# Seven block products for u in batches 3 to 6, relu in the gate, and kv loads issued after the spread of the roots

## The chip, the core and the metric

The kernel runs on one core of a Trainium2 chip. TensorE (PE) multiplies matrices, VectorE (DVE) and ScalarE (ACT) do the elementwise work, GpSimd (POOL) a little of it, and SyncE (SP) issues most of the transfers between HBM and the on-chip memory. Each engine works through its own list of instructions in order and is held by semaphores. The metric is the device time of one execution in microseconds (us).

## What is computed

Three layers follow one another, on 8 batches of 576 positions:

```python
kv = einsum('bhsd,bhse->bhde', k, v); out = einsum('bhsd,bhde->bhse', q, kv)      # 8 heads of 64
x = out / sqrt(mean(out*out) + 1e-6) * g_norm                                     # -> (8, 576, 512)
h = maximum(x @ w_in, 0); u, v = h[..., :512], h[..., 512:]
v_n = (v - mean(v)) / sqrt(var(v) + 1e-6)
gated = u * (einsum('ts,bsd->btd', w_spatial, v_n) + b_spatial)
y = gated @ w_out                                                                 # 512 -> 512
h = maximum(y @ w_in2, 0); c = conv over the positions, 3 taps per channel, of h  # 512 -> 1024
result = (h * sigmoid(c)) @ w_out2                                                # 1024 -> 512
```

## The kernel before

All matrices are fp32; a large product is made of three passes over operands that were split into a high part (rounded to fp32r) and a low part (the rest), so that each block of 128 rows of the contraction costs three matmuls. The program is written by hand, engine by engine; nothing schedules it. `w_out @ w_in2` is combined into one matrix at the start, so that y is never made. Two stages follow.

**Stage 1** (to about 408 us) has a body for each batch b. On PE its order is: the four tiles of v (`v_product`, L461, 12 matmuls of 512 columns each) and the rest tile (L487), between them the attention product o of batch b+1 (`o_product`, 16 matmuls); then the sum of squares for batch b+1 (`square_sum`), the kv product of batch b+2 (`kv_product`, L404), the product for u (`u_product`, L494: four output tiles m, each 2 x 12 matmuls of 288 columns), and the spatial product (`spatial_product`, L504: four tiles, each 28 matmuls of 288 columns). Every wait of PE is on a count of another engine's work: `s_vr` counts the relus of v (they free PSUM banks), `s_vlo` the low halves of the normalised v, `s_ur` the relus of u, `s_x` the split parts of the next batch's x, and `s_g` the gates. The tiles 0 and 1 of v of a batch start once three gates of the batch before are done (L467), the others after the fourth.

DVE's order in a body (`body`, L1138) is: for each of the five v tiles its statistics, scale and low part; a copy of half of kv; `inverse_root(b + 1)` (L1054), which makes the roots r of batch b+1 and ends at L1069; the last `v_lo`; `gate` 0 (L1133); `x_scale` of batch b+1 (L1071, four instructions); gate 1; `x_lo` (L1084, four and a rest); gate 2; gate 3; and four differences T of the gated values (`t_a`, `t_b`, `t_c`, L1185), which go to the operand scratch in HBM for stage 2. `x_scale` waits for `s_rB`.

SP sends the roots on their way (`spread_r`, L250): four small stores of r to HBM (L253), a wait for their landing, and two loads (L258) that spread them over all partitions into `rB` (sq_then_r in the trace). Then it waits for the kv product of batch b+2 and issues the load of k and v of batch b+3 (`load_kv`, L243), and then the stores of the gated values.

ACT does the relus (`v_relu`, `u_relu` L744), squares, square roots and high parts (`x_hi` L704, `v_hi`). In bodies 1 and 2 it also splits `w_out2`, and `wo2_store` (L818) sends the split half to HBM out of memory that it shares with stage 2.

**Stage 2** (from about 408 us) computes h in blocks by the scheme of seven products for a 2 x 2 block matrix product (`PRODUCTS`, L70), `in_product` (L608), with sums by DVE at L1285, and then the gate by the convolution and the last product.

Of the kernel before, what the change touches and what calls it, by code (L numbers as in the profile page):

```python
# [18 lines left out]
ALU = mybir.AluOpType  # L19
# [41 lines left out]

HI, LO = 0, 1
# [9 lines left out]
GROUPS = FT // 2  # L72
PER_BATCH = NPROD * GROUPS

# [6 lines left out]
def build(nc, q_T, kv_main_dram, kv_rest_dram, consts, w_in, w_sp_T, b_sp, w_out_T, w_in2, w_out2, wo2_dram, op_dram, r_dram, out):  # L81
    with ExitStack() as ctx:
# [104 lines left out]
        selT = sb("head_spread", [P, CH * MT, D])  # L187
# [36 lines left out]
        s_T, s_To = map(sem, ("s_T", "s_To"))  # L224
        s_go = [sem("s_go0"), sem("s_go1"), sem("s_go2")]
# [7 lines left out]
        s_odr = sem("s_odr")  # L233

# [7 lines left out]
        def _(sp):  # L242
# [78 lines left out]
            sp.wait_ge(s_u, B * MT)  # L321
# [81 lines left out]
        def _(pe):  # L403
# [100 lines left out]
            def spatial_product(b, m):  # L504
                if m == 0:
                    pe.wait_ge(s_vlo, (b + 1) * NT)
                    pe.wait_ge(s_ur, b * MT + 1)
                if m == 1:
                    pe.wait_ge(s_ur, b * MT + 2)
                if m == 2:  # L510
                    pe.wait_ge(s_ur, b * MT + 4)
# [3 lines left out]
                wide(GATE_PAIR[m], steps).then_inc(s_sp, 1)  # L515

            def body(b, ahead, two_ahead):
# [15 lines left out]
                for m in range(MT):  # L533
                    if m == 3 and two_ahead:
                        pe.wait_ge(s_kvd0, b + 3)
                        pe.wait_ge(s_kvd1, b + 3)
                    u_product(b, m, ahead)
# [3 lines left out]
                for m in range(MT):  # L541
                    spatial_product(b, m)
# [58 lines left out]
            body(0, True, True)  # L601
            with pe.Fori(1, B - 2) as b:
                body(b, True, True)
            body(B - 2, True, False)
            body(B - 1, False, False)

# [70 lines left out]
        def _(act):  # L677
# [26 lines left out]
            def x_hi(a, m):  # L704
                act.wait_ge(s_xm, a * MT + m + 1)
                if m == 0:
                    act.wait_ge(s_u, a * MT)
# [35 lines left out]

            def u_relu(b, m):  # L744
                act.wait_ge(s_u, b * MT + m + 1)
# [8 lines left out]
            def body(b, ahead, two_ahead):  # L754
# [18 lines left out]
                if two_ahead:  # L773
                    kv_copy(b + 2)
                u_relu(b, 0)
# [4 lines left out]
                if ahead:  # L780
# [9 lines left out]
                    for m in range(MT):  # L790
                        x_hi(b + 1, m)
                else:
# [111 lines left out]
            body(0, True, True)  # L904
            body(1, True, True)
            body(2, True, True)
# [559 lines left out]
```

## Time and profile before

| | us |
|---|---|
| median of 3 runs | 790.61 |
| lowest and highest run | 790.01, 791.25 |
| the profiled execution, its own time | 789.98 |
| its span in the trace | 788.0 |

Between the span and the own time of the profiled execution lie 2.0 us that the trace does not cover. The profile gives for every engine the busy time, for every group of instructions a mean duration, and for a wait who ended it. A row of the timeline has the start, the duration, the engine, the line of the source and the instruction, and in brackets the idle time ahead of it with what ended it. TensorE had its full clock in the whole span.

### The profile page before, as it was taken

The page shows a single profiled execution, that of the slowest core. Times are in us where ns is not written, and L with a number is a line of the kernel's source. Part 1 is how long each engine was busy: PE and PEld are TensorE (multiplying, and loading weights), DVE is VectorE, ACT ScalarE, POOL GpSimd, SP SyncE. Part 2 cuts the span into 40 slices and gives each one's busy share as a digit, 9 for nine tenths or more (in the row PEclk, how much of TensorE's full clock was granted, in tenths as well). Part 3 has the DMA queues.
Part 4 walks back from the last instruction along what each step waited for, and adds up shares of the span by engine and source line. Part 5 has one row for each costly group of instructions (what it writes and reads, how often), then busy time and mean ns, then how long its engine had stood idle before and what let it go on. Part 6 is the DMA issues. An engine that isn't in the chain of part 4 may idle for free.

```text
span 788.0 us, 15294 instructions
## 1 busy us (share of the span) xinstructions
PE 779.9 (99%) x5654; PEld 702.0 (89%) x5654; DVE 583.4 (74%) x1262; ACT 421.8 (54%) x753; POOL 29.4 (4%) x40
## 2 busy tenths in 40 slices
PE   9999999999999999999999999999999999999997
PEld 7679789798998979899999898998989899898986
DVE  3765785867577474757899989497985979689791
ACT  4664362644335253442457767375774757567562
POOL 4342000000000000000000000000000000000000
PEclk9999999999999999999999999999999999999999
DMA  9872629556252642213092212221021212102102
GB/s 325 306 254 67 245 92 296 208 193 233 76 209 86 195 150 61 106 46 99 23 364 74 106 42 105 68 104 56 7 109 58 105 53 101 57 14 105 54 0 67
DMA packets 35005, 96.92 MB, mean 123 GB/s; under 512 B 2738, under 2 KB 9106, under 8 KB 30228
## 3 DMA queue, kind: packets, MB, share of 16 engines
q1 hardware_dynamic: 33476, 90.09, 33.7%
q10 hardware_dynamic: 1488, 6.30, 2.1%
q8 instruction: 23, 0.38, 0.2%
q14 instruction: 18, 0.15, 0.1%
HBM read 66.11 MB, written 30.28 MB: 122 GB/s over the span
## 4 chain that ended last, share of the span: by engine, by line
PE 91%; DVE 3%; DMA 3%; ACT 1%; issue 1%; SPq 1%; ACTq 0%; DVEq 0%
PE ps L642 25%; PE ps L457 25%; PE ps L634 21%; PE ps L483 11%; PE ps L426 2%; PE ps L410 2%; PE ps L490 2%; PE ps L561 1%; DMA work<-w_out_T_dram 1%; DMA sq_then_r<-r_scratch 1%; PE ps L436 1%; DVE vrr L1115 0%; DVE h_and_sums L1285 0%; DVE t_then_s L1185 0%; PE ps L549 0%
## 5 line engine op out<-in xcount | busy, mean ns | idle before, releaser
L642 PE MATMUL ps<-w_in_split,v_hg_split 128*128 128x512 f32 x832 | 194.9, 390 | 0.0
L642 PEld LDWEIGHTS ps<-w_in_split,v_hg_split 128*128 128x128 f32 x832 | 155.7, 188 | 32.2
L457 PE MATMUL ps<-w_sp_split,v_hg_split 128*128 128x288 f32 x896 | 120.1, 295 | 0.0
L457 PEld LDWEIGHTS ps<-w_sp_split,v_hg_split 128*128 128x128 f32 x896 | 119.3, 188 | 0.0
L457 PE MATMUL ps<-x_operand_split,w_in_split 128*128 128x288 f32 x768 | 103.8, 296 | 0.0
L457 PEld LDWEIGHTS ps<-x_operand_split,w_in_split 128*128 128x128 f32 x768 | 102.1, 188 | 0.7 <-issue 0.2
L483 PE MATMUL ps<-w_in_split,x_operand_split 128*128 128x512 f32 x384 | 92.1, 393 | 1.6 <-DVE work L1136 1.6
L483 PEld LDWEIGHTS ps<-w_in_split,x_operand_split 128*128 128x128 f32 x384 | 71.1, 188 | 19.1 <-issue 3.1
L1285 DVE TENSOR_TENSOR h_and_sums<-h_and_sums,ps 128x288 f32<-128x288 f32 x160 | 68.4, 449 | 7.7 <-PE ps L634 7.2
L1136 DVE TENSOR_TENSOR work<-ps,work 128x576 f32<-128x576 f32 x32 | 24.0, 756 | 66.6 <-PE ps L457 66.5
L1285 DVE TENSOR_TENSOR h_and_sums<-work,ps 128x288 f32<-128x288 f32 x64 | 28.2, 450 | 46.8 <-PE ps L634 46.3
L634 PE MATMUL ps<-x_operand_split,w_combined 128*128 128x288 f32 x384 | 61.6, 295 | 0.0
L925 ACT ACTIVATE h_and_sums<-h_and_sums 128x576 f32<-128x576 f32 x64 | 43.4, 678 | 29.4 <-DVE h_and_sums L1285 28.7
L723 ACT ACTIVATE work<-ps 128x512 f32<-128x512 f32 x32 | 19.1, 597 | 74.1 <-PE ps L483 70.0
L634 PE MATMUL ps<-operand_more_split,w_combined_more 128*128 128x288 f32 x384 | 56.5, 295 | 0.3 <-DVE h_and_sums L1285 0.3
L634 PEld LDWEIGHTS ps<-x_operand_split,w_combined 128*128 128x128 f32 x384 | 54.7, 188 | 0.0
L634 PEld LDWEIGHTS ps<-operand_more_split,w_combined_more 128*128 128x128 f32 x384 | 52.9, 188 | 0.6 <-DVE h_and_sums L1285 0.6
L1328 DVE SCALAR_TENSOR_TENSOR work<-h_and_sums,const_cols,work 128x576 f32<-128x576 f32 x64 | 51.9, 812 | 0.3
L1322 DVE SCALAR_TENSOR_TENSOR work<-h_and_sums,const_cols,work 128x576 f32<-128x576 f32 x64 | 51.9, 811 | 0.0
L931 ACT ACTIVATE work<-h_and_sums,const_cols 128x576 f32<-128x576 f32 x64 | 49.7, 776 | 3.0
L1333 DVE TENSOR_TENSOR work<-h_and_sums,work 128x576 f32<-128x576 f32 x64 | 48.0, 750 | 0.3 <-ACT work L941 0.3
L752 ACT ACTIVATE work<-ps 128x576 f32<-128x576 f32 x32 | 20.8, 650 | 49.3 <-PE ps L457 49.2
(124 smaller groups left out, 1066.8 us busy)
## 6 DMA issues: line engine op xcount, KB each, us to landing
kv_raw<-kv_main_dram SPq DMA_DIRECT2D x8, 2048.0 KB, 11.8
q_raw<-q_T_dram SPq DMA_DIRECT2D x8, 1152.0 KB, 5.1
operand_scratch<-t_then_s SPq DMA_DIRECT2D x8, 1152.0 KB, 4.7
operand_raw<-operand_scratch SPq DMA_DIRECT2D x8, 1152.0 KB, 5.5
sq_then_r<-r_scratch SPq DMA_DIRECT2D x14, 576.0 KB, 7.0
operand_scratch<-work SPq DMA_DIRECT2D x24, 288.0 KB, 2.7
operand_more_raw<-operand_scratch SPq DMA_DIRECT2D x8, 864.0 KB, 7.2
w_out_split_scratch<-v_hg_split ACTq DMA_DIRECT2D x2, 2048.0 KB, 13.9
```

The lines of the kernel that those rows point to most:

```text
L457: last = pe.matmul(pair[bank][:, c, :], st, mo[:, c * HALF:(c + 1) * HALF], start=(n == 0), stop=(n == len(steps) - 1))
L483: last = pe.matmul(PS[:, V_BANK[i], 0:F1], XG[:, a, m, i * P:(i + 1) * P], WA[:, w, m, F1:2 * F1], start=(n == 0), stop=(n == len(steps) - 1))
L634: last = pe.matmul(PS[:, n % 8, 0:HALF], st, mo, start=(i == 0), stop=(i == len(steps) - 1))
L642: last = pe.matmul(PS[:, ROW_BANK[i], :], x, wout2[:, w, F_ORDER[e], :], start=(e == 0 and n == 0), stop=(e == FT - 1 and n == len(PASSES) ...
L752: act.activation(whole(u_sb[m]), pair[U_PAIR[m]], ACT.Relu).then_inc(s_ur, 1)
L925: act.activation(h_sb[f][:, 1:S + 1], h_sb[f][:, 1:S + 1], ACT.Relu).then_inc(s_hr, 1)
L931: act.activation(t_sb[e % 2], h_sb[f][:, 1:S + 1], ACT.Copy, scale=cols[:, FT + f:FT + f + 1]).then_inc(s_t0, 1)
L1136: dve.tensor_tensor(whole(u_sb[m]), pair[GATE_PAIR[m]], whole(u_sb[m]), ALU.mult).then_inc(s_g, 1)
L1285: dve.tensor_tensor(dst, x, PS[:, (g * NPROD + k) % 8, 0:HALF], ALU.add).then_inc(s_sum, 1)
L1322: dve.scalar_tensor_tensor(out=t, in0=h_sb[f][:, 0:S], scalar=cols[:, f:f + 1], in1=t, op0=ALU.mult, op1=ALU.add).then_inc(s_cv1, 1)
L1328: dve.scalar_tensor_tensor(out=t, in0=h_sb[f][:, 2:S + 2], scalar=cols[:, 2 * FT + f:2 * FT + f + 1], in1=t, op0=ALU.mult, op1=ALU.add).th ...
L1333: dve.tensor_tensor(p_sb[e % 2], h_sb[F_ORDER[e]][:, 1:S + 1], p_sb[e % 2], ALU.mult).then_inc(s_mul, 1)
```

## The change

Batches 3 to 6 (`FAST = 3` to B - 2) compute u in another way; batches 0, 1, 2 and 7 keep the eight block products.

- **PE.** `fast_product` takes the place of `u_product`: the 512 x 576 product is split into 2 x 2 blocks, and for each of two groups g seven products are made, each of 6 matmuls of 288 columns. That is 84 matmuls in place of 96. Product n waits for `s_vr` at n = 2, 3, 4, for the four operands T (`s_UTlo`) in group 0, and from n = 8 on for the sums of DVE that free its PSUM bank (`s_ux1`, `s_usum`).
- **DVE.** `u_sums` adds the products up: 7 additions of 128 x 288 for each group, after the last `v_lo`. `u_t_raw` makes four differences T of x of the next batch (128 x 576 each), ahead of gate 2; `u_t_lo` makes the low parts of the four (T2 and T1 ahead of gate 3, T3 after the first v tile and T4 after the last of the next body). `fast_gate` is `max(u, 0) * spatial` in one instruction; gate 0 stands behind `x_scale` in place of ahead of it. The first use of the T operands waits in body 2 for the landing of both stores of w_out2 (`s_wo2_st`), which lie in the same memory.
- **ACT.** The four `u_relu` of such a batch go; two `u_first_copy` (128 x 288) and four high parts `u_t_hi` come. The one of T4 stands ahead of the first copy.
- **Once.** `u_combine_weights` makes four combined weights: three instructions of 128 x 512 on DVE after `inverse_root(0)`, one after `kv_copy(1)`. Their high parts (ACT) and low parts (DVE) are made in body 1, the low parts ahead of gate 2.
- **SP.** In the bodies 0 to 4 a wait `s_rB` is put ahead of the load of k and v: it is issued only when both spread loads of the roots have landed. The loop over the batches is written out.

```diff
+            def fast_product(b, g, k, ahead, two_ahead):
+                n = g * NPROD + k
+                if n == 2:
+                    pe.wait_ge(s_vr, b * NT + 2)
+                elif n == 3:
+                    pe.wait_ge(s_vr, b * NT + 4)
+                elif n == 4:
+                    pe.wait_ge(s_vr, (b + 1) * NT)
...
+                elif n == 8:
+                    pe.wait_ge(s_ux1, b * U_GROUPS - FAST * U_GROUPS + 1)
+                elif n > 8:
+                    pe.wait_ge(s_usum, fast_u(b) + LAST_SUM[n - 8])
+                a, t = PRODUCTS[k]
+                if g == 0 and t in U_T_ORDER:
+                    pe.wait_ge(s_UTlo, fast_t(b) + U_T_ORDER.index(t) + 1)
...
-            with sp.Fori(0, B - 3) as b:
+            for b in range(B - 3):
                 sp.wait_ge(s_o, (b + 2) * MT)
                 load_q(b + 2)
                 spread_r(b + 1)
+                sp.wait_ge(s_rB, (b + 1) * CH * DMA)
                 sp.wait_ge(s_kv, b + 3)
                 load_kv(b + 3)
                 store_gated(b)
...
+                if isinstance(a, int) and a == FAST:
+                    dve.wait_ge(s_wo2_st, 2 * DMA)
...
+            def fast_gate(b, m):
+                if m == 0:
+                    dve.wait_ge(s_usum, fast_u(b) + U_PRODUCTS)
+                dve.wait_ge(s_sp, b * MT + m + 1)
+                dve.scalar_tensor_tensor(out=whole(u_sb[m]), in0=whole(u_sb[m]), scalar=0.0, in1=pair[FAST_GATE[m]],
+                                         op0=ALU.max, op1=ALU.mult).then_inc(s_g, 1)
...
+            def fast_body(b, two_ahead, make_t):
+                for i in range(NT):
+                    v_stats(b, i)
+                    if i == NT - 1:
+                        mean_square(b + 1)
+                    if i:
+                        v_lo(b, i - 1)
+                    v_normalise(b, i)
+                    if i == 0:
+                        u_t_lo(b, T3)
+                u_t_lo(b, T4)
+                if two_ahead:
+                    kv_copy(b + 2)
+                inverse_root(b + 1)
+                v_lo(b, NT - 1)
+                u_sums(b, 0)
+                u_sums(b, 1)
+                for m in range(MT):
+                    x_scale(b + 1, m)
+                fast_gate(b, 0)
+                for m in range(MT):
+                    x_lo(b + 1, m)
+                fast_gate(b, 1)
+                if make_t:
+                    u_t_raw(b + 1)
+                fast_gate(b, 2)
+                if make_t:
+                    u_t_lo(b + 1, T2)
+                    u_t_lo(b + 1, T1)
+                fast_gate(b, 3)
+                t_a(b)
+                t_b(b)
+                t_c(b)
```

On DVE, in the loop over the batches 3 to 5, this is what stands from the scaling of the next batch's x (o_x) to the end of the body. Before (work<-ps,work is a gate, t_then_s are the differences T for stage 2):

```order
L1136 TENSOR_TENSOR work<-ps,work 128x576
...
L1081 SCALAR_TENSOR_TENSOR o_x<-o_x,const_cols,sq_then_r 128x576 x4
...
L1136 TENSOR_TENSOR work<-ps,work 128x576
L1086 TENSOR_TENSOR x_operand_split<-o_x,x_operand_split 128x576 x4
L1089 TENSOR_TENSOR rest_split<-o_x,rest_split 128x4x64
...
L1136 TENSOR_TENSOR work<-ps,work 128x576
...
L1136 TENSOR_TENSOR work<-ps,work 128x576
...
L1185 TENSOR_TENSOR t_then_s<-work 128x576 x2
L1185 TENSOR_TENSOR t_then_s<-work,t_then_s 128x576 x2
```

Now (L1324 is a gate; w_out2_raw, the memory of the new operands T, is written at L1274, and their low parts at L1291):

```order
L1201 SCALAR_TENSOR_TENSOR o_x<-o_x,const_cols,sq_then_r 128x576 x4
...
L1324 SCALAR_TENSOR_TENSOR work<-work,ps 128x576
L1206 TENSOR_TENSOR x_operand_split<-o_x,x_operand_split 128x576 x4
L1209 TENSOR_TENSOR rest_split<-o_x,rest_split 128x4x64
...
L1324 SCALAR_TENSOR_TENSOR work<-work,ps 128x576
L1274 TENSOR_TENSOR w_out2_raw<-o_x 128x576
...
L1274 TENSOR_TENSOR w_out2_raw<-o_x,w_out2_raw 128x576
L1274 TENSOR_TENSOR w_out2_raw<-o_x 128x576
...
L1274 TENSOR_TENSOR w_out2_raw<-o_x,w_out2_raw 128x576
...
L1324 SCALAR_TENSOR_TENSOR work<-work,ps 128x576
L1291 TENSOR_TENSOR v_hg_split<-w_out2_raw,v_hg_split 128x576 x2
```

Gate 0 moved behind the scaling, and four differences stand between gates 1 and 2, two low parts between gates 2 and 3.

On DVE, from the making of the roots (r) to the scaling of x, batch 6 as it is written out. Before:

```order
L1069 TENSOR_TENSOR r<-r,std 128x144
L1129 TENSOR_TENSOR v_hg_split<-work,v_hg_split 128x512
L1136 TENSOR_TENSOR work<-ps,work 128x576
L1081 SCALAR_TENSOR_TENSOR o_x<-o_x,const_cols,sq_then_r 128x576 x4
L1136 TENSOR_TENSOR work<-ps,work 128x576
```

Now:

```order
L1189 TENSOR_TENSOR r<-r,std 128x144
L1249 TENSOR_TENSOR v_hg_split<-work,v_hg_split 128x512
L1295 TENSOR_TENSOR work<-work,ps 128x288 x14
L1201 SCALAR_TENSOR_TENSOR o_x<-o_x,const_cols,sq_then_r 128x576 x4
L1324 SCALAR_TENSOR_TENSOR work<-work,ps 128x576
```

The 14 sums of u came in between the last low part of v and the scaling.

## Rows read from the trace of the kernel before

**Rows 1.** The page, part 1: busy us, share of the span, instructions.

```profile
PE 779.9 (99%) x5654; PEld 702.0 (89%) x5654; DVE 583.4 (74%) x1262; ACT 421.8 (54%) x753; POOL 29.4 (4%) x40
```

**Rows 2.** Busy time per engine in stretches from one batch's start to the next.

```profile
136.08:182.88 46.80, 46.80 (x410) 42.20 (x409) 32.44 (x80) 21.39 (x41) 0.00 (x0) 1.00 0.65 220
...
229.67:276.46 46.79, 46.79 (x409) 42.18 (x409) 30.08 (x76) 19.44 (x37) 0.00 (x0) 1.00 0.44 145
...
323.26:367.56 44.30, 44.30 (x329) 39.77 (x329) 29.07 (x74) 18.64 (x35) 0.00 (x0) 1.00 0.25 75
```

**Rows 3.** Chain in order of time (start, us, what): batches 4 and 6.

```profile
248.69 27.77 PE ps L457 x208
...
339.80 27.77 PE ps L457 x208
```

**Rows 4.** Groups by line and form: xcount, busy us, mean ns, idle before.

```profile
L457 PE MATMUL ps<-w_sp_split,v_hg_split 128*128 128x288 f32 x896 | 120.1, 295 | 0.0
...
L1285 DVE TENSOR_TENSOR h_and_sums<-work,ps 128x288 f32<-128x288 f32 x64 | 28.2, 450 | 46.8 <-PE ps L634 46.3 <-ACT work L958 0.5
...
L1136 DVE TENSOR_TENSOR work<-ps,work 128x576 f32<-128x576 f32 x32 | 24.0, 756 | 66.6 <-PE ps L457 66.5
...
L1129 DVE TENSOR_TENSOR v_hg_split<-work,v_hg_split 128x512 fp32r<-128x512 f32 x32 | 21.9, 685 | 12.8 <-ACT v_hg_split L739 12.6
...
L1185 DVE TENSOR_TENSOR t_then_s<-work,t_then_s 128x576 f32<-128x576 f32 x16 | 12.1, 754 | 0.2
```

**Rows 5.** Timeline, DVE, batch 4.

```profile
229.78 0.76 DVE L1136 TENSOR_TENSOR work<-ps,work 128x576 f32<-128x576 f32 x1 [2.96 <-PE ps L457]
...
237.16 0.69 DVE L1102 BATCH_NORM_STATS2 bn_stats<-work 128x6 f32<-128x512 f32 x1 [0.89 <-ACT work L723]
...
241.84 0.69 DVE L1129 TENSOR_TENSOR v_hg_split<-work,v_hg_split 128x512 fp32r<-128x512 f32 x1 [0.56 <-ACT v_hg_split L739]
...
254.61 0.31 DVE L1069 TENSOR_TENSOR r<-r,std 128x144 f32<-128x144 f32 x1
...
266.10 3.00 DVE L1081 SCALAR_TENSOR_TENSOR o_x<-o_x,const_cols,sq_then_r 128x576 f32<-128x576 f32 x4
...
272.86 0.76 DVE L1136 TENSOR_TENSOR work<-ps,work 128x576 f32<-128x576 f32 x1
```

**Rows 6.** Timeline of batches 5 and 6: DVE, then SP, then DVE.

```profile
301.40 0.31 DVE L1069 TENSOR_TENSOR r<-r,std 128x144 f32<-128x144 f32 x1
...
305.02 1.21 SPq L258 DMA_DIRECT2D sq_then_r<-r_scratch  x2
...
347.14 0.31 DVE L1069 TENSOR_TENSOR r<-r,std 128x144 f32<-128x144 f32 x1
...
349.72 1.16 SPq L258 DMA_DIRECT2D sq_then_r<-r_scratch  x2
...
357.58 3.01 DVE L1081 SCALAR_TENSOR_TENSOR o_x<-o_x,const_cols,sq_then_r 128x576 f32<-128x576 f32 x4 [0.29 <-DMA sq_then_r<-r_scratch]
```

**Rows 7.** Timeline of batch 0 and the start of 1: DVE, then PE.

```profile
68.98 0.31 DVE L1069 TENSOR_TENSOR r<-r,std 128x144 f32<-128x144 f32 x1
...
81.60 3.00 DVE L1081 SCALAR_TENSOR_TENSOR o_x<-o_x,const_cols,sq_then_r 128x576 f32<-128x576 f32 x4 [4.45 <-DMA sq_then_r<-r_scratch]
...
89.00 3.03 PE L483 MATMUL ps<-w_in_split,x_operand_split 128*128 128x512 f32 x12 [1.57 <-DVE work L1136]
```

**Rows 8.** Timeline, DVE, batch 1: gate 2.

```profile
133.73 0.76 DVE L1136 TENSOR_TENSOR work<-ps,work 128x576 f32<-128x576 f32 x1
```

**Rows 9.** Batch 2: issue of the store, gate 2; time to landing.

```profile
168.07 0.33 ACTq L820 DMA_DIRECT2D w_out_split_scratch<-v_hg_split  x1
...
179.27 0.76 DVE L1136 TENSOR_TENSOR work<-ps,work 128x576 f32<-128x576 f32 x1
...
w_out_split_scratch<-v_hg_split ACTq DMA_DIRECT2D x1, 2048.0 KB, 13.2
```

**Rows 10.** Timeline, DVE, start-up.

```profile
31.59 1.54 DVE L1076 SCALAR_TENSOR_TENSOR o_x<-o_x,const_cols,ps 128x576 f32<-128x576 f32 x2 [2.51 <-PE ps L449]
```

More of the change, by code:

```diff
@@ L59, in ssq_bank @@
     return O_BANK[2] if isinstance(a, int) and a == 0 else SSQ_BANK
+FAST = 3
+FAST_BANK = [6, 7, 1, 0, 2, 3, 4, 5]
+FAST_GATE = [2, 3, 0, 1]
+HALF_D = F1 // 2
 HI, LO = 0, 1
@@ L233, in build, with plain_u, fast_u, fast_t @@
         s_odr = sem("s_odr")
+        def plain_u(b):
+            return FAST * MT if isinstance(b, int) and b == B - 1 else b * MT
+        def fast_u(b):
+            return b * U_PRODUCTS - FAST * U_PRODUCTS
+        def fast_t(b):
+            return b * 4 - FAST * 4
         def raw_weight(a):
@@ L532, in body @@
                     pe.wait_ge(s_winu, MT)
[L533 to L537, printed above, removed]
+                if fast:
+                    for g in range(U_GROUPS):
+                        for k in range(NPROD):
+                            fast_product(b, g, k, ahead, two_ahead)
+                else:
+                    for m in range(MT):
+                        if m == 3 and two_ahead:
+                            pe.wait_ge(s_kvd0, b + 3)
+                            pe.wait_ge(s_kvd1, b + 3)
+                        u_product(b, m, ahead)
                 if first:
@@ L774, in body @@
                     kv_copy(b + 2)
+                if fast:
+                    u_t_hi(b, T4)
+                    u_first_copy(b, 0)
+                    v_hi(b, NT - 1)
+                    u_first_copy(b, 1)
+                    for m in range(MT):
+                        x_hi(b + 1, m, True)
+                    if make_t:
+                        for t in U_T_ORDER[:3]:
+                            u_t_hi(b + 1, t)
+                    return
                 u_relu(b, 0)
@@ L791, in body @@
                         x_hi(b + 1, m)
+                    if isinstance(b, int) and b == 1:
+                        for n in range(4):
+                            u_weight_hi(n)
+                    if make_t:
+                        for t in U_T_ORDER[:3]:
+                            u_t_hi(b + 1, t)
                 else:
@@ new lines, in u_t_lo, with u_add, u_sums, own @@
+            def u_t_lo(a, t):
+                dve.wait_ge(s_UThi, fast_t(a) + U_T_ORDER.index(t) + 1)
+                dve.tensor_tensor(u_operand[t][LO], u_t_unsplit[t], u_operand[t][HI].bitcast(F32), ALU.subtract).then_inc(s_UTlo, 1)
+            def u_add(b, g, dst, x, k, product):
+                dve.wait_ge(s_up, fast_u(b) + g * NPROD + product + 1)
+                dve.tensor_tensor(dst, x, PS[:, FAST_BANK[(g * NPROD + k) % 8], 0:HALF], ALU.add).then_inc(s_usum, 1)
+            def u_sums(b, g):
+                def own(n):
+                    dve.wait_ge(s_usum, fast_u(b) + g * NPROD + n)
+                top, low = u_sb[g], u_sb[2 + g]
+                dve.wait_ge(s_ux1, b * U_GROUPS - FAST * U_GROUPS + g + 1)
+                if g:
+                    own(0)
+                else:
+                    for s in s_go:
+                        dve.wait_ge(s, DMA * b)
+                    dve.wait_ge(s_T, b * 4)
+                u_add(b, g, a_u2, a_x1, 1, 1)
+                u_add(b, g, top[:, 0:HALF], a_x1, 2, 2)
+                own(1)
+                u_add(b, g, a_u4, a_u2, 3, 3)
+                u_add(b, g, a_u3, a_u2, 5, 5)
+                own(3)
+                u_add(b, g, top[:, HALF:S], a_u4, 4, 5)
+                own(4)
+                u_add(b, g, low[:, HALF:S], a_u3, 3, 5)
+                u_add(b, g, low[:, 0:HALF], a_u3, 6, 6)
@@ L1167, in body @@
                         x_lo(b + 1, m)
+                    if isinstance(b, int) and b == 1:
+                        for n in range(4):
+                            u_weight_lo(n)
+                    if make_t:
+                        u_t_raw(b + 1)
                 else:
```

175 lines of the change are left out of this document (139 added, 36 removed).

## The prediction

> **What bounds the kernel now.** I read the busy times first: TensorE is busy 779.9 of 788.0 us, every other engine has room [rows 1]. So a matmul less is a gain, as long as nothing else comes to hold TensorE. Then the stretches of one batch each: 46.8 us, with TensorE busy in all of them and DVE in 30.08 of 46.79; in batch 6, which has no kv product left to make, 44.30 [rows 2]. The chain of work confirms it: in batch 4 u and the spatial product run without a gap as 208 matmuls in 27.77 us, 133.5 ns each [rows 3], though a single record reads 295 ns [rows 4], because matmuls overlap. The question is then what DVE does with its 16.7 idle us in a batch, and in what order.
>
> **The products saved.** 12 matmuls of 288 columns in each of four batches: 12 x 133.5 ns = 1.60 us, 6.4 us in all, if TensorE stays the bound.
>
> **What DVE gets.** In a batch 14 additions of 450 ns (the same instruction as in stage 2), and four differences and four low parts of 128 x 576 at about 754 ns [rows 4]: 6.3 + 6.0 = 12.3 us. With 30.1 that is 42.4 of a batch of 45.2. It fits as an average, but the order decides. I follow one loop, from the start of v in one batch to its start in the next.
>
> *From the start of v to the roots.* Batch 4 started at 229.67, and the last instruction of the roots ended at 254.92, 25.25 later [rows 2, 5]. Gate 3 began 0.1 after the start [rows 5]; now two low parts stand ahead of it, so that it and all behind it come about 1.1 later (an instruction of 754 ns lets the next one start some 0.08 earlier). T3's low part adds 0.67. Idle time of 0.89 and 0.56 [rows 5] takes up 1.45 of these 1.77; T4's low part comes behind it and adds 0.67. That makes 1.0 more: 26.25. Bounds: 0.7 (other small gaps give way too) and 1.3 (half of the 0.56 doesn't).
>
> *From the roots to the scaling.* The row for this is a batch whose DVE waited for the landing. In batch 6, with no kv load near it, the roots ended at 347.45 and scaling started at 357.58: 10.1 us [rows 6]. In batch 0, with the kv load issued behind the spread, it was 81.60 - 69.29 = 12.3 [rows 7]. In batch 5 the spread loads were issued 3.3 us after the roots (305.02 - 301.71), in batch 6 only 2.3 (349.72 - 347.45) [rows 6], so 11.1 is possible without the kv load. With that load behind it I take 10.5, near the lower end. In the kernel before, this landing was hidden: in batch 4 gate 0 was done only at 266.1, 11.2 after the roots [rows 5]. Now x_scale stands ahead of gate 0 and, as the sums end early, DVE waits for it.
>
> *From the scaling to the third gate.* Before, scaling started at 266.10 and gate 2 at 272.86, with one gate, x_lo and the rest between: 6.76 [rows 5]. Now gate 0 is in it too (0.7), then the four differences ahead of gate 2 (2.8 at their pace), then gate 2 itself (0.8): 11.1. TensorE may start v of the next batch only behind gate 2.
>
> The loop is 26.25 + 10.5 + 11.1 = 47.85 us, against 46.8 before. TensorE's own work would be 45.2. So **the loop through the spread becomes the bound**, and the 1.6 us saved are given back with 1.05 more, in three batches (3, 4, 5): +3.15. At the bounds (25.95 + 10.1 + 11.0, and 26.55 + 11.1 + 11.2) it is 0.25 to 2.05 for each batch.
>
> *The sums.* They start behind the last v_lo, at about 26.8 in the batch; the first is done at 27.25. TensorE starts u at 19.02 (248.69 - 229.67) [rows 2, 3] and would reach product 9, which waits for it, eight products of 0.80 us and one more later, at 26.2: 1.0 us of stall, then 0.3 at product 11, which waits for the sixth sum. In batches 3 to 5 this costs nothing on top, since the loop above is longer anyway; it shows what is late next.
>
> *Batch 6.* It makes no operands for batch 7, so the differences and two low parts are gone and the loop is short. But there is no kv product: u starts at 16.54 (339.80 - 323.26), 2.48 earlier, while the roots end at 24.19, only 1.06 earlier [rows 2, 3, 6]. The stalls at T4 and at the sums grow from 1.3 to 2.7. So 44.30 - 1.60 + 2.7: **+1.1**, with 0.6 and 1.6 as bounds.
>
> **Once.** *Batch 2.* The first four differences wait for the landing of the second w_out2 store: issued at 168.07, 13.2 us to landing, so 181.3; DVE would be ready at 179.3, where gate 2 stood [rows 9]. From 181.3 on: 2.8 for the differences and 0.9 for gate 2, 184.95, while v of batch 3 started at 182.88: +2.05. If the store lands by 179.3 it is +0.1. The kv load used to start at the same time as this store and now starts when the spread has landed, so the store may be quicker: I take **+1.4**.
>
> *Batch 1.* Four low parts of the weights, 685 ns each [rows 4], stand ahead of gate 2, which would end at 134.5 + 2.45 = 136.95 and not at 134.5 [rows 8]; v of batch 2 started at 136.08 [rows 2]. That is +0.9, or 0 if the spread lands earlier: **+0.3**.
>
> *Batch 0.* Here the spread was late, scaling waited 4.45 us, and TensorE stood still for 1.57 us behind gate 2 [rows 7]. With kv out of its way the landing could be up to 12.3 - 10.1 = 2.2 earlier: **-1.4**, bounds 0 and -1.57. This is the one part of the change from which I expect a gain.
>
> *Start-up.* Three combinations of weights (3 x 0.69) are behind the roots of batch 0, where DVE waited 2.51 us for TensorE [rows 10]: 0. The kv load still has more than 25 us to its product (rival 5); ACT loses four relus and was no bound; relu in the gate costs DVE 0.05 us. All 0.
>
> **Sum.** -1.4 + 0.3 + 1.4 + 3.15 + 1.1 = +4.55. On the profiled execution's own 789.98 (span 788.0 and 2.0 around it) that is 794.5; the median of the runs is 0.6 higher than it, so **795.1 us**. A measurement can tell about 0.2%, 1.6 us, from no change.
>
> **A rule against a row.** In batch 6 the two spread loads, 1.18 MB together, took from 349.72 to 357.58, 7.9 us from the first issue to the use [rows 6]. The Trainium skill, page "DMA: Bandwidth & Descriptors", section "Anatomy of one DMA — SWDGE (gpsimd) path", gives a transfer 2.0 us and its bytes at 436 GB/s; that would be an estimated 4.7 us here, 3.2 less, though its fit is for the other way of issuing, and this load reads the same rows of HBM for 64 partitions. By that rule the loop would be 44.7 and no bound, which is the second rival below. The trace does not agree, and no batch before shows a quicker landing.
>
> **The rivals.**
> 1. *The forecast*, the loop through the spread: 792.3 to 798.5. Chance 0.5.
> 2. *The spread lands early enough* (9 us or less after the roots, because nothing shares the queues with it): TensorE is the bound again, but still stalls 1.3 at the sums, so each batch gives 0.3 of its 1.6 us. -1.4 + 0.3 + 1.4 - 0.9 + 1.1 = +0.5: 791.1, no change. The same result comes from the lower bounds of all terms in the forecast (-1.5 + 0 + 0.1 + 0.75 + 0.6 = 0). Against it: batch 6 needed 10.1 with a free queue. Chance 0.2.
> 3. *The products come through*: landing early, and DVE's gaps swallow the low parts so that the sums are in time. -1.4 + 0.3 + 0.1 - 4.8 - 0.2 = -6: 784.6; half of it 788. For it: DVE's 16.7 idle us a batch. Against it: most of them lie in the second half of the batch, behind the roots, where they shorten nothing. Chance 0.12.
> 4. *It is worse*: DVE's chain to the roots has no gap to give and the spread takes 11.5 or more, because the stores of batch and operands share its time. Each 1 us costs 3 us in all: 799 to 802. It decides from a landing 11.5 after the roots. Chance 0.18.
> 5. *The kv load comes too late.* It starts some 8 us later, ahead of the scaling at about 37 us of the batch; its product stands 16 us into the next one, and the DMA engines are busy 0.44 of a batch [rows 2]. It decides from a load of over 25 us. Within the chance of 4.
>
> **Numbers.** Faster by over 0.2%: case 3 and the edge of case 2, 0.14. Within 0.2%: the rest of case 2 and the low edge of the forecast, 0.21. Slower: 0.65. The range 789.0 to 799.5 leaves out most of case 3 and the end of case 4.
>
> **What would show it.** In the trace of the changed kernel: DVE waiting 3 to 5 us for the spread ahead of x_scale in batches 3 to 5, and TensorE waiting 2 to 3 us at the start of v for the third gate; stretches of 47.5 to 48.2 from batch 3 to 6; waits of TensorE for the sums of about 1 us, more in batch 6, where T4 holds it too; a wait of DVE for the w_out2 store in batch 2; in batch 1 no wait at the start any more. I am wrong if x_scale starts without a wait, or if stretches of 45.2 to 45.7 stand there: then the landing or DVE's way to the roots is shorter than the rows of before say.

## The result

The changed kernel takes 792.33 us (median of 21 runs, 791.45 to 794.57) against 790.61 (21 runs of the kernel before): the ratio is 1.0023, 95% interval 1.0016 to 1.0031. It is slower by 1.8 us, 1.3 to 2.5 at the ends of the interval. The direction was forecast, the size was not: +4.5 us were forecast, +1.8 came. The profiled execution took 791.45 us with a span of 789.6, against 789.98 and 788.0.

The page of the changed kernel, part 1, answers to [rows 1]:

```profile
PE 776.1 (98%) x5606; PEld 695.4 (88%) x5606; DVE 632.7 (80%) x1358; ACT 426.8 (54%) x765; POOL 30.2 (4%) x40
```

TensorE is busy 3.8 us less (48 matmuls fewer; 6.4 us were forecast), DVE 49.3 more. Part 4, the chain of work that ended last, shows whose turn it was, first before, then in the changed kernel:

```profile
PE 91%; DVE 3%; DMA 3%; ACT 1%; issue 1%; SPq 1%; ACTq 0%; DVEq 0%
```

```profile
PE 74%; DVE 14%; DMA 4%; issue 4%; ACT 2%; SPq 1%; DVEq 0%; ACTq 0%
```

TensorE held 91% of that chain before; now DVE and transfers have taken part of it. The timeline of batch 4 shows where, and it answers to [rows 5]: DVE from the end of the roots to the third gate (start, us, line and instruction, in brackets the idle time ahead and what ended it), and then TensorE:

```profile
254.73 0.31 DVE L1189 TENSOR_TENSOR r<-r,std 128x144 f32<-128x144 f32 x1
...
265.17 3.00 DVE L1201 SCALAR_TENSOR_TENSOR o_x<-o_x,const_cols,sq_then_r 128x576 f32<-128x576 f32 x4 [3.71 <-DMA sq_then_r<-r_scratch]
...
271.76 0.75 DVE L1324 SCALAR_TENSOR_TENSOR work<-work,ps 128x576 f32<-128x576 f32 x1
...
274.56 0.75 DVE L1274 TENSOR_TENSOR w_out_raw<-o_x,w_out_raw 128x576 f32<-128x576 f32 x1
275.23 0.75 DVE L1324 SCALAR_TENSOR_TENSOR work<-work,ps 128x576 f32<-128x576 f32 x1
...
256.19 1.06 PE L571 MATMUL ps<-x_operand_split,w_in_split 128*128 128x288 f32 x6 [0.89 <-DVE work L1295]
...
276.03 3.00 PE L528 MATMUL ps<-w_in_split,x_operand_split 128*128 128x512 f32 x12 [0.51 <-DVE work L1324]
```

The roots end at 255.04, 26.34 after the start of v at 228.70; DVE waits 3.71 us for the landing and starts scaling 10.13 after the roots; gate 2 ends at 275.98 and TensorE starts v of batch 5 at 276.03, after a wait of its own of 0.51. The stretches, from the first matmul of v in one batch to that in the next, in the two traces:

| stretch | before | after | difference | forecast |
|---|---|---|---|---|
| start to batch 0 | 40.36 | 40.56 | +0.20 | 0 |
| batch 0 | 48.64 | 46.91 | -1.73 | -1.4 |
| batch 1 | 46.92 | 46.81 | -0.11 | +0.3 |
| batch 2 | 46.79 | 46.93 | +0.14 | +1.4 |
| batches 3, 4, 5 | 140.38 | 142.35 | +1.97 | +3.15 |
| batch 6 | 44.31 | 45.38 | +1.07 | +1.1 |
| batch 7 and stage 2 | 420.60 | 420.66 | +0.06 | 0 |
| span | 788.0 | 789.6 | +1.6 | +4.55 |

The differences of two single executions at the start are noise of this size: the first matmul of v lay between 39.93 and 41.33 in all profiled runs of this study.

Two more rows of the changed kernel. The store of w_out2 in batch 2, time from issue to landing, against the 13.2 of [rows 9], and the first T block with gate 2 on DVE there:

```profile
w_out_split_scratch<-v_hg_split ACTq DMA_DIRECT2D x1, 2048.0 KB, 8.1
...
177.60 0.75 DVE L1274 TENSOR_TENSOR w_out_raw<-o_x 128x576 f32<-128x576 f32 x1
...
180.40 0.75 DVE L1330 TENSOR_TENSOR work<-ps,work 128x576 f32<-128x576 f32 x1
```

It landed after 8.1 us, before DVE was ready for it, so nothing waited. The order of the issues had turned round. Before, the kv load was issued 2.4 us ahead of this store (at 165.67, the store at 168.07 in [rows 9]); now it comes 3.4 us behind it:

```profile
165.67 0.59 SPq L244 DMA_DIRECT2D kv_raw<-kv_main_dram  x1
```

```profile
166.43 0.33 ACTq L940 DMA_DIRECT2D w_out_split_scratch<-v_hg_split  x1
...
169.80 0.60 SPq L288 DMA_DIRECT2D kv_raw<-kv_main_dram  x1
```

What was forecast and did not come: TensorE waits 0.51 to 0.70 us at the start of v and not 2 to 3, and DVE does not wait for the w_out2 store.

### The profile page after: what moved, and what is told of

The parts are those of the page before. It is cut to its first block, busy times and chain, and to the rows that moved or that the text cites. A ratio compares the mean times of both kernels' runs of the same rounds, so it can differ in the third digit from the quotient of the medians.

```text
span 789.6 us, 15258 instructions
## 1 busy us (share of the span) xinstructions
PE 776.1 (98%) x5606; PEld 695.4 (88%) x5606; DVE 632.7 (80%) x1358; ACT 426.8 (54%) x765; POOL 30.2 (4%) x40
## 4 chain that ended last, share of the span: by engine, by line
PE 74%; DVE 14%; DMA 4%; issue 4%; ACT 2%; SPq 1%; DVEq 0%; ACTq 0%
PE ps L726 25%; PE ps L718 21%; PE ps L502 15%; PE ps L528 6%; DMA sq_then_r<-r_scratch 3%; PE ps L455 2%; PE ps L643 1%; DVE t_then_s L1421 1%; DVE bn_stats L1222 1%; DVE x_operand_split L1206 1%; DVE o_x L1201 1%; PE ps L471 1%; PE ps L631 1%; PE ps L535 1%; DVE v_hg_split L1291 1%
## 5 line engine op out<-in xcount | busy, mean ns | idle before, releaser
L1523 DVE TENSOR_TENSOR h_and_sums<-work,ps 128x288 f32<-128x288 f32 x64 | 28.3, 451 | 46.7 <-PE ps L718 46.2
L795 ACT ACTIVATE x_operand_split<-o_x 128x576 fp32r<-128x576 f32 x32 | 21.8, 686 | 57.1 <-DVE o_x L1201 53.8
L502 PE MATMUL ps<-x_operand_split,w_in_split 128*128 128x288 f32 x384 | 51.8, 295 | 0.0
L502 PEld LDWEIGHTS ps<-x_operand_split,w_in_split 128*128 128x128 f32 x384 | 51.1, 188 | 0.3
L1061 ACT ACTIVATE work<-work 128x576 f32<-128x576 f32 x64 | 43.6, 681 | 2.3 <-DVE work L1566 1.8
```

The costliest lines, as they stand in the source:

```text
L502: last = pe.matmul(pair[bank][:, c, :], st, mo[:, c * HALF:(c + 1) * HALF], start=(n == 0), stop=(n == len(steps) - 1))
L795: act.activation(XG[:, HI, m, :], o_T[:, m, :], ACT.Copy).then_inc(s_xhi, 1)
L1061: act.activation(p_sb[e % 2], t_sb[e % 2], ACT.Sigmoid).then_inc(s_sig, 1)
L1523: dve.tensor_tensor(dst, x, PS[:, (g * NPROD + k) % 8, 0:HALF], ALU.add).then_inc(s_sum, 1)
```

## The experiments

Ratios are to the kernel before, whose runs each group shares. "The loop" is the way from the roots of one batch over the landed spread and everything that DVE then does to the roots of the next.

### The kv load at once (only that part undone)

```diff
-                sp.wait_ge(s_rB, (b + 1) * CH * DMA)
                 sp.wait_ge(s_kv, b + 3)
                 load_kv(b + 3)
```

> The changed kernel (792.3 us, 1.0023 of before) without the wait for s_rB ahead of the kv load: only that part of the change is undone. My theory: the move of the kv load is worth what batch 0 and batch 2 gained. The spread of batch 0 lands late again and TensorE stands still at the start of batch 1 (+1.6 to 1.9 us), and the w_out2 store of batch 2, which landed 8.1 us after its issue with the kv load behind the spread and 13.2 us before, lands late again, so that the four differences hold gate 2 (+1.9 us by the sum of the prediction). The loop of batches 3 to 5 gets 0 to 0.5 us longer each. Sum +3.5 to +5.3: 795.8 to 797.6, ratio to before 1.0068 to 1.0090. Rival (the place of the kv load is neutral, the gain of batch 0 has another cause, such as the loop on SP being written out): 792.3, ratio 1.002.

Measured: 795.69 us, ratio 1.0076 (1.0061 to 1.0091): the ratio is in the expected band, but not by the expected terms. The store, time to landing, and the start of v in batches 1 and 3:

```profile
w_out_split_scratch<-v_hg_split ACTq DMA_DIRECT2D x1, 2048.0 KB, 12.7
...
88.54 3.00 PE L527 MATMUL ps<-w_in_split,x_operand_split 128*128 128x512 f32 x12
...
184.05 2.99 PE L527 MATMUL ps<-w_in_split,x_operand_split 128*128 128x512 f32 x12 [1.53 <-DVE work L1329]
```

With the kv load ahead of it the store takes 12.7 us again and holds gate 2: TensorE waits 1.53 us and the stretch of batch 2 is 48.58 (184.05 - 135.47), 1.65 more than in the changed kernel. That is near the price which the prediction set for it (+2.05 with a landing after 13.2). The stretch of batch 3 is 0.54 longer too, batches 4 and 5 are not. But the start of batch 1 comes at 88.54 - 41.33 = 47.21 after the first v, 0.30 later than in the changed kernel, not 1.6 to 1.9. So the stall of batch 0 did not come back, and its end had another cause. These differences add up to 2.6 us of the 3.3 by which the span is longer; the rest lies ahead of the first v.

### The kernel before with the late kv load

```diff
-            with sp.Fori(0, B - 3) as b:
+            for b in range(B - 3):
...
+                sp.wait_ge(s_rB, (b + 1) * CH * DMA)
```

> The kernel before with the other part of the change alone: the kv load waits for the landed spread, and the loop on SP is written out. My theory: the stall of TensorE at the start of batch 1 (1.57 us and the slow first tile behind it) goes and nothing else changes, since batches 1 to 7 were bound by TensorE: -1.6 to -1.9 us, 788.7 to 789.0, ratio 0.9977 to 0.9980. Rival (the kv load comes too late for its product or holds the stores of the operands): 790.6 or more, ratio 1.000 or above.

Measured: 788.83 us, ratio 0.9983 (0.9974 to 0.9991). The stretch of batch 0 is 46.91, as in the changed kernel. The number was right; that it came from the kv load was still only assumed, since this edit has two parts. This run is also the fair partner of the changed kernel, which has both parts too: against it (0.9983 and 1.0023) the seven products with all that they bring cost 3.2 us and not 1.8.

### The kernel before with the loop on SP written out, and nothing else

```diff
-            with sp.Fori(0, B - 3) as b:
+            for b in range(B - 3):
```

> The kernel before with the loop over the batches on SP written out and the kv load left where it was. It splits the gain of batch 0 (from the stretch of 48.64 us from the first v to that of batch 1 to 46.91). In the run with the kv load at once that stretch was 47.21, so by theory the written-out loop alone (issues of the roots in 1.3 us in place of 1.7, and the first of them sooner) gives about 1.4 of the 1.7 us: 789.2, ratio 0.998. Rival (the late kv load gives it all): 790.6, ratio 1.000, stretch 48.6. If the first holds, the gain that the prediction gave to the late kv load belongs to the loop on SP.

Measured: 788.83 us, ratio 0.9980 (0.9971 to 0.9990). This one line gives all of the gain that the two parts give together (0.9983). The queue of SP in batch 0, first the kernel before, then this one:

```profile
69.47 1.71 SPq L253 DMA_DIRECT2D r_scratch<-r  x4
72.11 1.75 SPq L258 DMA_DIRECT2D sq_then_r<-r_scratch  x2
74.13 0.58 SPq L244 DMA_DIRECT2D kv_raw<-kv_main_dram  x1
```

```profile
70.12 1.29 SPq L253 DMA_DIRECT2D r_scratch<-r  x4
72.35 1.12 SPq L258 DMA_DIRECT2D sq_then_r<-r_scratch  x2
73.51 1.08 SPq L244 DMA_DIRECT2D kv_raw<-kv_main_dram  x1
```

Before, the roots ended at 69.29, the first store was issued 0.18 later, the four took 1.71 and the two spread loads 1.75: the second was in the queue at 73.86, 4.6 after the roots. Written out, the roots end at 70.09, the first issue follows in 0.03, the four take 1.29 and the two 1.12: in the queue at 73.47, 3.4 after the roots. The scaling of x starts 10.6 us after the roots (80.69 - 70.09) in place of 12.3, and TensorE's start of batch 1 is no longer late (88.09 - 41.14 = 46.95). The issue accounts for 1.2 of the 1.7 us; where the other 0.5 come from is not shown.

Why the issue is quicker is open. That the loop's register makes each transfer dearer would be the obvious reason, but the spread of batch 5 is issued behind the loop in the kernel before, and it took 1.71 for the four stores as well. With the loop written out the same instructions take 1.29 and the loads follow sooner. First before, then this run:

```profile
301.74 1.71 SPq L253 DMA_DIRECT2D r_scratch<-r  x4
305.02 1.21 SPq L258 DMA_DIRECT2D sq_then_r<-r_scratch  x2
```

```profile
300.81 1.29 SPq L253 DMA_DIRECT2D r_scratch<-r  x4
303.04 1.14 SPq L258 DMA_DIRECT2D sq_then_r<-r_scratch  x2
```

### Half of the spread

```diff
-                    rows = r_dram[a, c].rearrange("m s -> (m s)").partition_broadcast(D)
+                    rows = r_dram[a, c, 0:2].rearrange("m s -> (m s)").partition_broadcast(D)
```

> The changed kernel with the two loads that spread the roots cut to half of their bytes (output tiles m = 0 and 1 only; the scaling of x in the tiles 2 and 3 is left without its roots). Theory A (batches 3 to 5 are bound by a loop through the landing of the spread: roots, 10.13 us, scaling and all that follows on DVE to the next roots): the landing comes about 2 us earlier, about 8.1 us after the roots, DVE waits about 1.7 us where it waited 3.7, and the stretches of batches 3 to 5 fall from 47.4 to about 46.1, where TensorE (45.2 and 0.9 of waits for the sums) is the bound: -3 to -4 us in all, 788.5 to 789.3, ratio 0.9975 to 0.998. Theory B (TensorE is held by the waits for the sums and by slow restarts, the landing is no bound): the stretches stay at 47.4, 792.3, ratio 1.002.

This kernel leaves two of the four output tiles without their roots. Measured: 788.20 us, ratio 0.9977 (0.9967 to 0.9986), as theory A says. Who waited for whom on DVE, batches 3 to 6 (us in total, times, longest), after and here:

```profile
DVE o_x L1201 <- DMA sq_then_r<-r_scratch: 15.4, 4, 4.1
```

```profile
DVE work L1324 <- PE ps L502: 7.9, 5, 3.0
DVE o_x L1201 <- DMA sq_then_r<-r_scratch: 4.0, 4, 1.2
```

The wait for the landing falls from 15.4 to 4.0 us, and DVE now waits for TensorE's spatial product instead, 7.9 us. The scaling starts 7.1 us after the roots in batch 4 (260.39 - 253.29), the stretches of batches 3 to 5 are 46.65, 46.40 and 46.41. The landing came 1 us earlier than theory A said (7.1 and not 8.1), but TensorE held the batch at 46.4 and not at 46.1. Theory B falls.

### The differences T behind gate 2

```diff
                 fast_gate(b, 1)
+                fast_gate(b, 2)
                 if make_t:
                     u_t_raw(b + 1)
-                fast_gate(b, 2)
-                if make_t:
                     u_t_lo(b + 1, T2)
```

> The changed kernel with the four differences T of x put behind gate 2 in batches 3 to 5 (body 2 stays as it is). In the prediction the loop ran through TensorE's start of v, which waits for gate 2. Theory A1 (that is so): gate 2 comes 2.8 us earlier, TensorE starts v without a wait, the stretches fall from 47.4 to 46.1 to 46.6: -2.4 to -3.9 us in all, ratio 0.9974 to 0.9993. Theory A2 (the loop is DVE's alone: it is never idle from the scaling to the next roots but for latencies, so the roots come no earlier, whatever TensorE's start does): TensorE starts v at most 0.5 to 0.7 us earlier and then waits for the sums by as much more; stretches stay at 47.2 to 47.4, total 791.8 to 792.3, ratio 1.0015 to 1.0023.

Measured: 792.60 us, ratio 1.0032 (1.0021 to 1.0043): no gain. TensorE starts v of the next batch without a wait for gate 2 now, but in batches 4 and 5 its waits for the sums of u grow from 0.9 to 1.6 us (first the changed kernel, then this one, all waits of batches 3 to 6):

```profile
PE ps L571 <- DVE work L1295: 3.2, 4, 0.9
PE ps L528 <- DVE work L1324: 1.9, 3, 0.7
```

```profile
PE ps L571 <- DVE work L1295: 4.5, 4, 1.6
```

The roots of batches 3, 4 and 5 end at 207.52, 254.83 and 302.11, 47.3 apart as in the changed kernel (207.56, 255.04, 302.38). So in these batches TensorE's start is not a node of the loop: it is DVE's and the spread's alone. In batch 6 TensorE waits 2.42 us at T4 in place of 1.33, so what it won at the starts is given back there:

```profile
346.52 1.83 PE L571 MATMUL ps<-x_operand_split,w_in_split 128*128 128x288 f32 x12 [2.42 <-DVE x_operand_split L1291]
```

The granted clock stays at 1.00 behind this wait (third number from the right in the row of the stretch):

```profile
346.50:350.00 3.50, 2.95 (x20) 2.74 (x21) 3.36 (x9) 0.00 (x0) 0.00 (x0) 1.00 0.01 3
```

### Gate 0 ahead of the scaling

```diff
-                for m in range(MT):
-                    x_scale(b + 1, m)
                 fast_gate(b, 0)
+                for m in range(MT):
+                    x_scale(b + 1, m)
```

> The changed kernel (792.3 us, 1.0023) with gate 0 back ahead of the scaling of x in batches 3 to 6, as it stood before. By the loop that is DVE's and the spread's alone: in batch 4 the spatial tile 0 is ready at 264.5 and the landing at 265.1, so gate 0 fits into the wait for the landing and its 0.67 us leave the loop: stretches from 47.4 to 46.7, -2.0 us in all, 790.3, ratio 0.9997. Rival (the order of DVE's list is neutral, its whole load is the bound): 792.3, 1.0023. Second rival (gate 0 is ready only after the landing and delays the scaling): 792.3 or above.

Measured: 790.13 us, ratio 0.9995 (0.9986 to 1.0004), the 2 us expected. The roots are 46.9 and 46.7 apart (207.63, 254.57, 301.24).

### The kv copy behind the roots

```diff
-                if two_ahead:
-                    kv_copy(b + 2)
                 inverse_root(b + 1)
+                if two_ahead:
+                    kv_copy(b + 2)
                 v_lo(b, NT - 1)
```

> The changed kernel with DVE's half of the kv copy put behind the roots in batches 3 to 5. By the loop: the roots end 0.9 us earlier and the landing follows; DVE waits 3.7 us there, so the copy costs nothing in its new place. The loop falls from 47.4 to 46.5; TensorE waits up to 0.7 us for the copy at product 7 but as much less at the sums, so it is bound at about 46.4, the stretch of the run with half a spread. -2.7 us in all, 789.6, ratio 0.9989. Rival (product 7 and the sums both hold TensorE, the gain is eaten): 791.5 to 792.3, ratio 1.001 to 1.002.

Measured: 789.33 us, ratio 0.9983 (0.9973 to 0.9993). Stretches of 46.86, 46.63 and 46.57. TensorE waits for the copy, as expected at product 7, and for nothing at the sums behind it:

```profile
PE ps L571 <- DVE kv_double L1161: 3.7, 3, 1.3
...
PE ps L571 <- DVE work L1295: 0.5, 1, 0.5
```

The 0.5 at the sums is that of batch 6. The wait is 1.3, not 0.7: there the loop is no bound any more, TensorE is.

### Two more instructions on DVE, in two places

```diff
+                for i in (0, 1):
+                    dve.bn_stats(spare[:, i * 6:(i + 1) * 6], W[:, 0, 0, 0, :])
```

> The changed kernel with two more instructions on DVE (statistics of 128 x 512 into a spare tile, some 0.62 us each) in every one of batches 3 to 6, put where DVE waits for the landing of the spread, behind the sums. If the place decides: the wait falls from 3.7 to about 2.4 us and the time stays, 792.3, ratio 1.002. If DVE's load as such is the bound: +1.2 us a batch, 796 to 797, ratio 1.008.

> The changed kernel with the same two instructions on DVE in batches 3 to 6, put behind gate 1. If the place decides: here they are in the loop, stretches of 48.6 in place of 47.4 in batches 3 to 5, and up to 1 us in batch 6: +3.6 to 4.8 us, 795.9 to 797.1, ratio 1.007 to 1.0085. If DVE's load as such is the bound it is the same as with the instructions in the wait; if neither, 792.3.

Measured in the wait: 792.45 us, ratio 1.0026 (1.0016 to 1.0036), no change from 1.0023. The waits for the landing are 10.5 us in place of 15.4:

```profile
DVE o_x L1202 <- DMA sq_then_r<-r_scratch: 10.5, 4, 2.7
```

Measured behind gate 1: 798.77 us, ratio 1.0089 (1.0065 to 1.0114), more than the 795.9 to 797.1 expected. The same 1.2 us of work costs nothing in the one place and about 6 us in all in the other (by the medians; 5 by the ratios). The stretch of batch 3 is 48.64, as expected (48.6). Those of batches 4 and 5 are 50.20 and 50.09, and their roots come 50.1 us apart in place of 47.4, 2.7 more and not 1.2. TensorE starts v behind a wait of 1.82, 1.89 and 1.89 us in batches 4, 5 and 6. The rows of the last two, and the stretches around them (window and length, busy us and count of PE, weight load, DVE, ACT and POOL; then the granted clock, 1.00 is full, the DMA share and GB/s):

```profile
280.52 4.55 PE L529 MATMUL ps<-w_in_split,x_operand_split 128*128 128x512 f32 x12 [1.89 <-DVE work L1325]
...
330.61 2.96 PE L529 MATMUL ps<-w_in_split,x_operand_split 128*128 128x512 f32 x12 [1.89 <-DVE work L1325]
```

```profile
277.00:280.50 3.50, 1.63 (x13) 1.40 (x11) 3.47 (x7) 1.92 (x3) 0.00 (x0) 1.00 0.28 91
280.50:285.10 4.60, 4.58 (x16) 3.17 (x20) 4.46 (x7) 0.02 (x1) 0.00 (x0) 0.63 0.31 111
285.10:290.00 4.90, 4.90 (x33) 3.62 (x34) 3.54 (x12) 4.05 (x8) 0.00 (x0) 1.00 0.68 257
330.60:333.60 3.00, 2.99 (x16) 2.26 (x20) 2.90 (x5) 0.00 (x0) 0.00 (x0) 1.00 0.00 0
```

In batch 5 the 12 matmuls behind the wait take 4.55 us in place of 3.00 in the changed kernel: the granted clock is 1.00 up to the wait, 0.63 in the 4.6 us behind it and 1.00 again after that, so a part of the tile ran at the lower level (1.2 GHz) and a part at the full one (2.4 GHz). Batch 4 has the same (4.61 us for the tile). The v tile, its statistics and the roots come 1.5 us later by that, which is the rest of the 2.7; here TensorE's start is on the loop after all. In batch 6 the wait is as long, 1.89, and the clock stays at 1.00. The runs differ in it too: one took 794.88 at a mean granted clock of 1.000, the other three 798.6 to 799.0 at 0.994 to 0.996.

### All three orders together

```diff
                 u_t_lo(b, T4)
-                if two_ahead:
-                    kv_copy(b + 2)
                 inverse_root(b + 1)
-                v_lo(b, NT - 1)
+                if two_ahead:
+                    kv_copy(b + 2)
                 u_sums(b, 0)
+                v_lo(b, NT - 1)
                 u_sums(b, 1)
+                fast_gate(b, 0)
                 for m in range(MT):
                     x_scale(b + 1, m)
-                fast_gate(b, 0)
```

> The changed kernel with three changes of order on DVE in batches 3 to 6: the kv copy behind the roots, gate 0 ahead of the scaling, the last v_lo behind the first seven sums of u. By the loop: 47.4 - 0.9 - 0.67 = 45.8 us for it, and TensorE, held at 46.6 by the kv copy at product 7 and by the sums, is the bound; with the v_lo behind the first seven sums these are 0.6 us earlier, but product 7 still waits 1.2 us for the kv copy. Stretches of 46.4 in batches 3 to 5 and 44.7 in batch 6: -3 to -4 us against the changed kernel, 788.3 to 789.3, ratio to before 0.9975 to 0.999. Rival (the gains of the orders add up, the product 7 doesn't hold): 45.8 a batch, 787.0, ratio 0.996.

Measured: 789.05 us, ratio 0.9986 (0.9976 to 0.9995). The time lies in the band of the first version (788.3 to 789.3), but the stretches do not: they are 46.86, 46.82 and 46.81 in place of 46.4 (or 45.8 by the rival). The scaling waits for no landing any more in batches 3 to 5. By the waits that are left, what binds now is a chain without the spread: v, the roots, the copy of kv, product 7, the rest of u and the spatial product (no run took a link out of it). TensorE waits 1.3 us at product 7 in each of batches 3 to 5, and at T4 in batch 6:

```profile
PE ps L571 <- DVE kv_double L1161: 4.0, 3, 1.3
PE ps L571 <- DVE x_operand_split L1291: 1.4, 1, 1.4
```

So the seven products give a batch of 46.8 us, what it had with eight, and batch 6 is 44.87 in place of 44.31. The gain over the kernel before, 1.1 us, is no larger than the 1.6 that the written-out loop on SP gives alone; the intervals of the two overlap. In the traces batches 3 to 6 together are 0.7 us longer here than in the kernel before with that loop written out. The lowest median of a version that computes everything is that kernel's, 788.83 us (788.83 with the late kv load too).

## Why the prediction was right and wrong

**The step that failed.** The mechanism came, the size of the sum did not, +1.8 us in place of +4.5. Two terms were mis-sized above all: the loss of 1.05 us a batch in the loop through the spread, which measured 0.66 on average, and the +1.4 for the wait on the w_out2 store in batch 2, which measured +0.14. In the loop it was the landing of the spread, taken as 10.5 us after the roots and measured as 10.1 to 10.3, and the way from the scaling to gate 2, taken as 11.1 and measured as 10.8. And the prediction had TensorE's start of v as a link of the loop, with a wait of 2 to 3 us; the wait was 0.51 to 0.70.

**The bound moves to the loop through the spread: right.** Half a spread took 4 us away, work in the wait cost nothing, the same work behind it cost at least its length. The three terms of the loop were 26.25, 10.5 and 11.1; batch 4 measured 26.34, 10.13 and 10.86, together 47.33 in place of 47.85. The 1.05 us lost per batch were mis-sized because the small term is the difference of large ones: in batches 3, 4 and 5 it was 0.70, 0.53 and 0.74. The landing came out near the lower bound, the 10.1 of batch 6: 10.27, 10.13 and 10.22. With the loop on SP written out, the spread loads are issued 2.3 us after the roots, as in batch 6 before; in batch 4 it was 2.8 before. I had seen such a difference in batch 5 (3.3 against 2.3 us) and took a value between the two; the one line of the diff takes it away (303.04 - 300.78 = 2.26 in the run with that line alone), though by what means is not shown. This term is 1.2 us of the 2.95 that the sum was too high. The prediction read its starts of v from the chain of work, where they lie 0.16 us behind the first matmul of the timeline (229.67 against 229.51), so that its loop left out about 0.2 us; without that slip the sum would have been farther off.

**The products saved: half of the 1.60 us.** TensorE's busy time in a batch fell from 46.79 to 45.93, and in batch 6 from 44.30 to 43.53:

```profile
228.70:276.03 47.33, 45.93 (x396) 40.67 (x396) 40.51 (x99) 20.11 (x39) 0.00 (x0) 1.00 0.45 144
323.56:368.94 45.38, 43.53 (x316) 38.34 (x317) 36.56 (x92) 17.47 (x34) 0.00 (x0) 1.00 0.24 73
```

The idle time of batch 4 is 1.40 us, 0.51 at the start and 0.89 at the sums. The other 0.7 against the 45.2 of the prediction are no idle time in the rows: a cut in the row of matmuls costs more than the wait. The spatial product fills 15.02 us ahead of a wait, where 14.85 pass if v follows at once (261.45 to 276.30 in the kernel before), and the first product behind the sums takes 0.89 us (256.19 to 257.08) in place of 0.79. Pieces of this kind make up most of the 0.7. In batches 3 to 5 this changes nothing, since the loop is longer; it is why TensorE could not fall to 45.2 in the run with half a spread either (46.40, of it 45.70 busy).

**Which chain it is: wrong in one node.** I let the loop run through TensorE's start of v behind gate 2, and so expected it to wait 2 to 3 us there. The run with T behind gate 2 shows that DVE's list closes it alone. A reader who had acted on my version would have moved gate 2 and gained nothing; what helps is to take work out from between the landing and the next roots (gate 0, the kv copy).

**Batch 2: the term of the sum that was most mis-sized.** +1.4 was forecast for the wait on the w_out2 store, +0.14 measured. Both bounds were named (0.1 and 2.05) and I took a value between them, nearer to the old landing. The reason for the lower bound, that the kv load now starts later than this store, was stated and then given too little weight: the store took 8.1 us with the kv load behind it and 12.7 with the kv load ahead of it. That is 1.3 us of the 2.95.

**Batch 1:** forecast +0.3, measured -0.11. The scaling waited 1.33 us for its landing before and did not wait after (it starts at 124.09, right behind gate 0), so the low parts of the weights found room, and behind the stall at the start of batch 1 a little more had been lost than the wait itself. 0.4 of the 2.95.

**Batch 0:** forecast -1.4, measured -1.73. The size was nearly right, the cause was wrong: not the kv load out of the spread's way but the written-out loop on SP. In the prediction the line of the diff on this loop has no term at all.

**Batch 6:** +1.1 forecast, +1.07 measured, with the waits named, 1.33 at T4 and 0.52 at the sums. That the number fits is in part luck: the waits are 1.85 and not 2.7, and the matmuls gave 0.8 and not 1.6. **The sums:** 1.0 us at product 9 forecast, 0.87 to 0.89 measured in the three batches.

**The rivals.** The spread that lands within 9 us (rival 2) did not come: 7.9 us from the first spread issue to use were seen before, and 7.86 in batch 4 after (265.17 - 257.31). By the Trainium skill, page "DMA: Bandwidth & Descriptors", section "Anatomy of one DMA — SWDGE (gpsimd) path", the two loads would take an estimated 4.7 us, though its fit is for another way of issuing than these loads have. The measured 7.86 do not agree. The late kv load (rival 5) did no harm. The time that came, 792.33, lies on the edge that I had put between the forecast and rival 2 (792.3), and it came there by the forecast's mechanism with sizes near its lower bounds. That it is the one and not the other is shown by the runs, not by the number.

## What to carry to other kernels

Work that is saved on the engine that is the bound is worth no more than the next chain allows, and a chain that was hidden for many microseconds (here the 10 us from the roots to their landed spread) can become the bound as soon as DVE does more in front of it and behind it. Before moving instructions, find which events close the loop from one iteration to the next: only what stands between the landing and the next issue counts, and what stands in the wait is free as long as it fits into it. When an edit has a side line, such as a loop written out, give it its own term and its own run.

## What the runs showed of the hardware

- **The same issues took less time with SP's loop written out.** In batch 0 four stores of the roots took 1.71 us in the loop and 1.29 written out; with the two loads behind them the spread was in the queue 1.2 us sooner. Stores issued just behind the loop took 1.71 as well, so the cause is open. It is the one-line edit that made the kernel before 1.6 us faster.
- **The clock fell behind some waits of TensorE, and their length did not decide it.** In one trace it fell behind waits of 1.82 and 1.89 us (tiles of v of 4.61 and 4.55 us, granted clock 0.63 behind the second) and stayed at 1.00 behind another of 1.89 (2.96 us). In the run with T behind gate 2 it stayed at 1.00 behind a wait of 2.42. Behind all waits of 0.5 to 1.6 us in these traces it stayed too; the tile of v then took 3.0 us against 2.9 without a wait. What else decides it, no run here varied.
- **Two large transfers on two queues slow each other, and it matters which is issued first.** The 2 MB store took 12.7 to 13.2 us to landing with the kv load issued 2.4 to 3.3 us ahead of it (three traces), and 8.1 to 8.5 with the kv load issued 3.4 us behind it (two traces). The kv load of the same batch took 16.9 us before and 10.1 in the changed kernel, so in the new order both are quicker; there it also starts only when the spread has landed.
- **The spread was slowed less by a kv load right behind it.** In the run that issues the kv load at once the scaling started 10.83, 10.26 (268.68 - 258.42) and 10.17 us after the roots in batches 3, 4 and 5, against 10.27, 10.13 and 10.22 in the changed kernel, where the kv load waits for the landing.
